# Attention scores from rounded parts: three single-pass products on row halves in place of one fp32 product, the first pair of heads left as it was

## The reference, cut to what matters

```python
# q, k, v: (4, 8, 1152, 64) fp32; w_in: (512, 2048), w_out: (2048, 512), alpha: (2048,)
q_pool = q.reshape(B, H, S // 2, 2, D).mean(axis=3)          # 576 queries a head
scores = scale * np.matmul(q_pool, k.transpose(0, 1, 3, 2))  # 576 x 1152
scores = scores - np.max(scores, axis=-1, keepdims=True)
attn = np.exp(scores)
attn = attn / (np.sum(attn, axis=-1, keepdims=True) + 1e-09)
out = np.matmul(attn, v)
...
x = out.transpose(0, 2, 1, 3).reshape(B * S, H * D)          # 2304 x 512
h = x @ w_in
g = np.maximum(h, 0.0) + alpha * np.minimum(h, 0.0)
return g @ w_out
```

## Time and profile before

| | us |
|---|---|
| median of 3 runs | 889.04 (888.99 to 889.9) |
| the profiled execution | 888.61 |
| span of its core, first to last instruction | 886.8 |

### The profile page before, as it was taken

One profiled execution on the slowest core, in us unless ns is written; L12 is line 12 of the kernel. 1 busy time (PEld: TensorE's weight loads), 2 busy tenths in 40 slices (PEclk: granted clock), 3 DMA queues, 4 the chain that ended last, 5 costly groups with the idle time before them and its releaser, 6 DMA issues. The chain is left out here.

```text
span 886.8 us, 20078 instructions
## 1 busy us (share of the span) xinstructions
PE 861.6 (97%) x6631; PEld 618.1 (70%) x6631; DVE 514.7 (58%) x792; ACT 422.4 (48%) x935; POOL 204.8 (23%) x170
## 2 busy tenths in 40 slices
PE   8899999999999999999999999999999999999997
PEld 5455555555555555555557999998999998999996
DVE  4677777777777777777674344444434445444443
ACT  3666666666666666666663222225222224222222
POOL 3101111110101111110403322333223323233230
PEclk9999999999999999999999999999999999999999
DMA  8725644464435634464122212123222222321211
GB/s 196 174 58 135 152 94 115 97 152 116 122 95 125 152 94 111 101 152 113 48 86 69 60 59 71 59 60 107 84 70 61 59 66 88 109 59 59 63 43 72
DMA packets 42670, 84.37 MB, mean 95 GB/s; under 512 B 7568, under 2 KB 15760, under 8 KB 42640
## 3 DMA queue, kind: packets, MB, share of 16 engines
q1 hardware_dynamic: 40640, 80.06, 35.2%
q10 hardware_dynamic: 2000, 3.93, 1.3%
HBM read 79.18 MB, written 4.79 MB: 95 GB/s over the span
## 5 line engine op out<-in xcount | busy, mean ns | idle before, releaser
L763 PE MATMUL slot_ps<-ff 128*128 128x384 f32 x1152 | 217.8, 337 | 1.4 <-PEq L760 1.4
L763 PEld LDWEIGHTS slot_ps<-ff 128*128 128x128 f32 x1152 | 204.3, 188 | 11.1 <-issue 3.3
L546 DVE TENSOR_REDUCE neg_max<-s_ps 128x1 f32<-128x1152 f32 x144 | 194.7, 1352 | 18.1 <-DVEq L545 17.4
L779 PE MATMUL s_ps<-ff 128*128 128x512 f32 x720 | 182.3, 394 | 1.7 <-PEq L777 1.3
L677 PE MATMUL s_ps<-k_f,q_f 64*128 64x512 f32 (+1 forms) x640 | 159.2, 620 | 1.3 <-PEq L729 1.1
L443 ACT ACTIVATE e_sb<-s_ps,neg_max 128x1024 f32<-128x1024 f32 x144 | 159.6, 1109 | 0.0
L710 PE MATMUL pv_ps<-pt,v_f 128*64 128x256 f32 (+1 forms) x1152 | 155.1, 412 | 0.2 <-PEq L729 0.2
L779 PEld LDWEIGHTS s_ps<-ff 128*128 128x128 f32 x720 | 133.4, 188 | 26.0 <-issue 3.0
L710 PEld LDWEIGHTS pv_ps<-pt,v_f 128*64 128x64 f32 x1152 | 76.7, 136 | 95.9 <-issue 52.6
L598 DVE TENSOR_SCALAR e_sb<-slot_ps,alpha_sb 128x384 f32<-128x384 f32 x96 | 59.3, 617 | 113.2 <-DVEq L596 113.2
L580 DVE COPY pt<-slot_ps 128x512 f32<-128x512 f32 x144 | 98.6, 685 | 39.1 <-DVEq L579 39.1
(11 more groups left out here) (47 smaller groups left out, 525.6 us busy)
## 6 DMA issues: line engine op xcount, KB each, us to landing
k_f<-in_k SPq DMA_DIRECT2D x64, 288.0 KB, 4.2
q_raw<-in_q SPq DMA_DIRECT2D x62, 288.0 KB, 4.1
wi_raw<-in_w_in SPq DMA_DIRECT2D x48, 256.0 KB, 2.6
wo_raw<-in_w_out SPq DMA_DIRECT2D x48, 256.0 KB, 2.6
v_f<-in_v SPq DMA_DIRECT2D x32, 288.0 KB, 3.7
out<-pt ACTq DMA_DIRECT2D x5, 768.0 KB, 4.1
inv_bc<-sums SPq DMA_DIRECT2D x32, 80.0 KB, 3.7
k_end<-in_k SPq DMA_DIRECT2D x64, 32.0 KB, 3.9
```

The costliest lines, as they stand in the source:

```text
L546: nc.vector.tensor_reduce(out=neg_max[:, b:b + 1], in_=s_ps[:, S_AT[b]:S_AT[b] + NKEY], op=ALU.max, axis=AX_X, negate=True).then_inc(max_r ...
L763: ins = nc.tensor.matmul(slot_ps[h][:, 0:TOK], w[i][:, d * P:(d + 1) * P], x[h][:, d * TOK:(d + 1) * TOK], start=(d == 0 and w is wi_hi an ...
L779: ins = nc.tensor.matmul(y_ps[h][t], g[h][:, t * P:(t + 1) * P], w[i], start=(first == 0 and j == 0), stop=(last == 1 and j == 2))
```

## The change

From the second pair of heads on, the large scores are made as the feed-forward products are: q and k are each split into a rounded part and the rest, and the scores are the sum of q_hi k_hi, q_hi k_lo and q_lo k_hi, accumulated in PSUM, each product again as two matmuls on the two row halves. The mixed tile has six such products: the queries get 64 columns of zeros, put in on the host (`with_gaps`), so that 128 columns of the first head end in zeros and 128 of the second begin with them, and both add up in one tile. The small scores stay fp32. The first pair of heads keeps the fp32 scores (`first_scores`); its raw q and k lie at the end of `x_f`, in the part that is written last.

k no longer goes straight into its place: it is loaded into one raw buffer, and GpSimd makes from it k_hi, k_lo and k_end, and from q the pooled q_f, q_hi and q_lo. The parts of even pairs and of odd pairs are two halves of one tensor `kq`, which also takes the place of `ff` in the feed-forward half; so GpSimd waits for the last release of the even set before it splits x. A pair's buffers are released by one semaphore, `qk_free`. SyncE's queue has another order.

```diff
-                for h, first, m, to in SOURCE[t]:
...
             def big_scores(s):
 
-                t, b, g = s % TILES, s % 2, s // TILES % 2
+                b, g = s % 2, s // TILES % 2
+                terms = []
+                for h, col in WIDE[s % TILES]:
+                    i = 2 * g + h
+                    terms += [(q_hi[i], k_hi[i], col), (q_hi[i], k_lo[i], col), (q_lo[i], k_hi[i], col)]
+                pieces = [None, None]
+                for j, (qp, kp, col) in enumerate(terms):
+                    for row, at in enumerate(BIG[b]):
+                        rows = slice(row * HALF, (row + 1) * HALF)
+                        pieces[row] = nc.tensor.matmul(s_ps[:, S_AT[b] + at:S_AT[b] + at + BANK],
+                                                       qp[rows, col:col + P], kp[rows, at:at + BANK],
+                                                       start=(j == 0), stop=(j == len(terms) - 1))
+                return pieces
...
-                    for ins in big_scores(s + 2):
+                    for ins in first_scores(s + 2) if s + 2 < TILES else big_scores(s + 2):
                         ins.then_inc(s_ready, 1)
...
+            def split_q(i, raw, done):
...
+                nc.gpsimd.tensor_copy(q_hi[i], q_f[i][:, :]).then_inc(pool_self, 1)
+                pool.wait_ge(pool_self, 1).then_inc(pool_self, -1)
+                nc.gpsimd.tensor_tensor(q_lo[i], q_f[i][:, :], q_hi[i].bitcast(F32),
+                                        ALU.subtract).then_inc(pool_self, 1)
...
+            def split_qk(i):
+                split_q(i, q_raw, q_raw_in)
                 pool.sem_inc(q_raw_free, 1)
...
+                pool.wait_ge(k_raw_in, 32).then_inc(k_raw_in, -32)
+                nc.gpsimd.tensor_copy(k_hi[i], k_raw[:, :]).then_inc(pool_self, 1)
+                pool.wait_ge(pool_self, 1).then_inc(pool_self, -1)
+                nc.gpsimd.tensor_tensor(k_lo[i], k_raw[:, :], k_hi[i].bitcast(F32), ALU.subtract).then_inc(pool_self, 1)
+                pool.wait_ge(pool_self, 1).then_inc(pool_self, -1)
+                nc.gpsimd.tensor_copy(k_end[i][0:D, :, :], key_ends(k_raw[0:D, :])).then_inc(pool_self, 1)
+                pool.wait_ge(pool_self, 1).then_inc(pool_self, -1)
+                pool.sem_inc(k_ready[i], 1)
+                pool.sem_inc(k_raw_free, 1)
+
+            def split_pair(g):
+                pool.wait_ge(qk_free[g], 1).then_inc(qk_free[g], -1)
+                split_qk(2 * g), split_qk(2 * g + 1)
...
             pool.wait_ge(x_done, NPAIR - 2)
+            pool.wait_ge(qk_free[0], 1).then_inc(qk_free[0], -1)
...
             with sp.Fori(0, NPAIR // 2 - 2) as two:
                 for g in range(2):
 
-                    sums_and_qk(two * 2 + 3 + g, 1 - g)
+                    store_sums(0), spread_sums(0)
+                    load_q_raw(two * 4 + 7 + 2 * g)
+                    store_sums(1)
+                    load_k_raw(two * 4 + 7 + 2 * g)
+                    spread_sums(1)
                     load_v_pair(two * 2 + 2 + g, g)
+                    load_qk(two * 4 + 8 + 2 * g)
...
+    def with_gaps(a):
+
+        gap = np.zeros(a[0::2].shape[:3] + (P // 2,), a.dtype)
+        first, second = a[0::2], a[1::2]
+        both = np.stack((np.concatenate((first[..., :320], gap, first[..., 320:]), axis=3),
+                         np.concatenate((gap, second), axis=3)), axis=1)
+        return both.reshape((a.shape[0],) + both.shape[2:])
```

More of the change, by code:

```diff
@@ L127, in build @@
                 [s_ps[:, 3 * BANK:4 * BANK], s_ps[:, 4 * BANK:5 * BANK], pv_ps[:, :]]]
-        k_in = [sem(f"k{i}_in") for i in range(4)]
+        k_raw_in = sem("k_raw_in")
+        q_raw_in = sem("q_raw_in")
         k_upper_in = [sem(f"k{i}_upper_in") for i in range(2)]
@@ L147, in build @@
         q_ready = [sem(f"q{i}_ready") for i in range(4)]
+        k_ready = [sem(f"k{i}_ready") for i in range(4)]
         pool_self = sem("pool_self")
@@ L663, in small_scores @@
                 rows = UPPER if s < 4 else slice(0, P)
-                for h, first, m, to in SOURCE[t]:
+                for h, col, m, to in SOURCE[t]:
                     ins = nc.tensor.matmul(s_ps[to:to + m, S_AT[b] + at:S_AT[b] + at + P],
-                                           q_f[2 * g + h][rows, first:first + m], k_end[2 * g + h][rows, end, :],
+                                           q_f[2 * g + h][rows, col:col + m], k_end[2 * g + h][rows, end, :],
                                            start=True, stop=True)
@@ L675, in big_scores @@
                     rows = slice(row * HALF, (row + 1) * HALF) if s > 1 else UPPER
-                    for h, first, m, to in SOURCE[t]:
+                    for h, col, m, to in SOURCE[s]:
                         ins = nc.tensor.matmul(s_ps[to:to + m, S_AT[b] + at:S_AT[b] + at + BANK],
-                                               q_f[2 * g + h][rows, first:first + m],
-                                               k_f[2 * g + h][rows, at:at + BANK], start=True, stop=True)
+                                               q_f[h][rows, col:col + m], k_first[h][rows, at:at + BANK],
+                                               start=True, stop=True)
                     pieces.append(ins)
@@ L692, in begin_scores @@
                     i = 2 * g + t
-                    pe.wait_ge(k_in[i], 64).then_inc(k_in[i], -64)
+                    pe.wait_ge(k_ready[i], 1).then_inc(k_ready[i], -1)
                     pe.wait_ge(q_ready[i], 1).then_inc(q_ready[i], -1)
@@ L797, in _ @@
             small_scores(0).then_inc(bank2_ready, 1)
-            for ins in big_scores(0):
+            for ins in first_scores(0):
                 ins.then_inc(s_ready, 1)
@@ L801, in _ @@
             begin_scores(1)
-            for ins in big_scores(1):
+            for ins in first_scores(1):
                 ins.then_inc(s_ready, 1)
```

148 lines of the change are left out of this document (78 added, 70 removed).

## The result

| | before | after |
|---|---|---|
| median, us | 889.1 (888.99 to 889.9, 4 runs) | 893.36 (893.22 to 893.66, 4 runs) |
| span of the profiled core, us | 886.8 | 891.5 |

The changed kernel is slower: 1.0049 times the time of before, 95% interval 1.0036 to 1.0061. The forecast was 888.7, no change that can be measured; the range of 881 to 903 holds the time.

A forecast was written before the change was run, and what follows sets the result against it. TensorE, 97% busy, was taken to bound only four of nine attention stretches, waiting for the ring in the others. Bursts -1.7, first tiles +0.2 and VectorE holds +1.2 gave -0.3: 888.7 us against 889.04, range 881 to 903.

The forecast's parts named there:

- SyncE's queue: Loads and stores of sums: a store slipping by a microsecond leaves reciprocals wanted only 12 us after it; cost nothing.
- 0 to 3 us; I take 0: GpSimd's work at the start, before the burst of step 8: if late, a one-time cost; taken as 0.
- Rival 4: GpSimd or a transfer is late for a head, each pair, needing 6 us more than reckoned; 895; chance 0.04.
- Bursts: TensorE's large scores: plain bursts fall from 1.01 to 0.85 us, mixed ones rise from 1.02 and 1.24 to 1.55.
- rival 3: TensorE's pair of passes is dearer than 0.232, for instance through unhidden weight loading; 893 to about 912; chance 0.14.
- What reaches the end: Attention loop: shorter bursts count only in four of nine stretches, mixed tiles cost 0.84 a body; net -1.7 us.
- the ring: Attention half: ninth copy, row maximum and cut exponential on VectorE and ScalarE, starting from TensorE's small scores; TensorE waits for it.
- VectorE against GpSimd: Invert of group 1 meets GpSimd's rounding of k, waiting 0.1 to 0.2 us; half of +2.4 taken, +1.2.
- Rival 2: Group 1's invert meets GpSimd's subtraction of k, holding VectorE up to 2.6 us once a pair; 922; chance 0.08.
- GpSimd: Seven instructions a head in place of two, 21 to 22 us a pair; hidden, by 6 us.
- The start: GpSimd's and VectorE's q work on the first tiles grows by 64 columns; +0.2 us.

The follow-up runs named there:

- Experiments 1 to 3: Changed kernel with the second group's store earlier (891.36 us); with it one transfer later (900.54); the first of these with even heads' k loads also behind the store (888.48).
- experiment 5: Changed kernel with the second group's store earlier, its large scores made from the rounded parts' product alone; 895.10 us, ratio 1.0081.
- experiment 8: Changed kernel with four raw k buffers, SyncE's queue ordered as before the change, and mixed-tile scores in fp32; 933.61 us, ratio 1.0530.
- experiment 3: Changed kernel with the second group's store earlier and each even head's k load moved behind the first group's store; 888.48 us, ratio 0.9995.
- experiment 2: Changed kernel with the second group's store put one transfer later, behind the load of head 6's q; 900.54 us, ratio 1.0126.

## Why the prediction was wrong, point by point

**The step that failed is "SyncE's queue", its "Nothing" for the store of the sums.** It looked at the loop, where the store is due 22 us after the release and the reciprocals have 12 us in hand, and not at the instructions ahead of the loop, where two heads' loads stand in front of the same store and each k waits for GpSimd. There the store slipped not by a microsecond but by 9.5, and with the 7.7 us of the way through DRAM (55.47 to 63.22) that is more than the 14 until VectorE is ready for the reciprocals (45.97 to 60.11). Experiments 1 to 3 give it its price: by the profile 3.4 us of waiting and 2.1 of a lower clock at the first place; by the medians 2.0 for the first alone and 2.9 more for the second, which takes the first one's place once that is gone; 4.9 in all. The clue was in the diff and in the prediction's own numbers: two heads are 21 us of GpSimd, and the line `load_qk(4), load_qk(5)` stands ahead of `store_sums(1)`. The prediction reckoned GpSimd's lateness at the start ("0 to 3 us; I take 0") only as far as the burst of step 8 that needs the parts, not as far as the loads, and what is queued behind them. Rival 4 named a late GpSimd or transfer, each pair, at 895; it came once, and cost nearly as much.

**Bursts.** Forecast 0.85 and 1.55, measured 0.87 and 1.57 to 1.59. The pair of passes came out as forecast, 0.23 for 0.232: the second to the fifth pair of a mixed burst start 0.69 apart. What the prediction had too small, by some 0.02, is the fixed part for filling and changing over, 0.155. The two row halves run side by side, and rival 3 falls. The Trainium skill's page "TensorE: Matmul & The Clock Gate", Part 3, says that a load overlaps running matmuls only when the row group differs. The trace is at odds with it: from 226.50 on each weight load (0.18) starts with the matmul of its own half and is done before the next pair, 0.23 later.

**What reaches the end.** Forecast -1.7 us for 7.5 bodies, -0.23 a body; measured -0.22 a body over the six from step 34 to 142. The split under it holds in its direction: over the same six bodies the kernel with fp32 mixed tiles gains 4.5 us more than the one beside it, 0.75 a body, where the longer mixed bursts are 0.9 and the prediction charged 0.84. That leaves 0.97 a body that the plain bursts save, of 16 x 0.14 = 2.2: under half, where the prediction's -1.7 us holds 1.07. So added length cost some 0.8 of itself and removed length gave back 0.4; that a longer burst pushes the ring where a shorter one waits for it is a reading of these two numbers that no run tests by itself.

**Luck in the total.** With the two places repaired the kernel stands at -0.7 against the kernel before, near the forecast of -0.3, but partly by chance: the forecast holds +1.2 for holds of VectorE in the loop that cost nothing, and leaves out what the start costs, below.

**VectorE against GpSimd.** The prediction took +1.2 for an invert that would have to wait 0.1 to 0.2 in the rounding of k. The phase came out as reckoned, within 0.1: in the changed kernel's loop the sum starts 0.06 to 0.14 before the rounding ends. The cost was nothing: a held sum ends some 0.02 after GpSimd's instruction, and one that starts 0.13 or less before that end is done by then in its usual 0.15. Rival 2 did not happen but its mechanism is shown, at up to its price: 2.25 us in experiment 5, at the invert of group 1 that it named, and 2.43 in experiment 8, at the invert of group 0, because GpSimd was late and not early. The sum of row_sum ends with GpSimd's instruction, whether that has two inputs (1.14, 2.43) or one (0.64). The Trainium skill's page "SBUF — State Buffer", in the section on the two separate sides, has an exclusive lock in both directions, and the trace agrees with this rule; the prediction's doubt whether VectorE could be held is settled.

**GpSimd** takes from 215.04 to 236.04 for a pair, 21.0, as reckoned.

**The start.** Forecast +0.2, measured +0.5 at step 1 (17.14 against 16.61), but the other kernels with the same start, experiment 3's among them, were 0.0 to 0.9 late there in their profiled executions. Whether the change costs anything in these first steps stays open.

**The first pass through the ring.** From the start of step 10 to that of step 12 the changed kernel loses 0.87, which is in the 0.8 of step 14 and was not in the sum. Half of it is the first mixed tile in the new form: step 11 costs 0.43 in the changed kernel and in every run with the same bursts, and nothing in the two with fp32 mixed tiles. The rest, 0.44 in step 10, is for the most part VectorE held ahead of the loop, where the prediction looked for no such wait:

```profile
45.07 0.42 DVE L606 SCALAR_TENSOR_TENSOR sum_eps<-row_sum 128x4 f32<-128x4 f32 x1
```

```profile
43.93 1.55 POOL L391 TENSOR_TENSOR q_raw<-q_raw 128x640 f32<-128x640 f32 x1 [3.90 <-POOLq L390]
```

The sum lasts 0.27 too long. In experiment 3's kernel the same one lasts 1.08, and step 10 loses 1.10; with four buffers for raw k it is not held, and step 10 loses 0.16.

## What to carry to other kernels

When a load gets a new condition, walk the queue that issues it from its first instruction, not only through the loop's steady state: ahead of the loop the consumers are not yet in phase, and one wait in the wrong place costs once what no later step gives back. After a gap is closed, look again at the next one behind it; it may have been hidden by the first. In a kernel that is bound by a ring through several engines, price longer and shorter work apart: here what was added to a burst counted for some 0.8 of its length and what was taken away for less than half. And when less work gives no less time, look on the other engines for an instruction that lasts longer than it did.

## What the runs showed of the hardware

- VectorE's scalar_tensor_tensor on 128x4 with both inputs in SBUF waits for a running GpSimd instruction to end, also when that has one input: 1.14 and 0.64 us for what takes 0.15 alone. A VectorE reciprocal with one input did not wait (0.18), and a sum that began 0.08 before GpSimd's end still took 0.15.
- With one product in place of two the time rose from 882.96 to 895.10: TensorE's gaps of 1.7 to 3.9 us came behind held sums of 0.98 to 3.19, and the granted clock fell behind five of the eight, to 0.50 behind the longest two. Gaps of nearly one length differ in this: behind those of 1.8 that end at 163.31 and 219.48 the clock fell, behind those that end at 108.00, 335.55 and 390.64 it stayed at 1.00.
- After an idle gap of 3.2 us the clock stayed at 0.50 in the rows of the next five us, all of it work, and then came back; that cost 2.1 us more on top of the gap, and 2.0 behind the gap of 10.4 us of experiment 2.
- A pair of fp32r passes over 512 columns, one on each row half, takes 0.23 us, as one such pass on the whole array did in the feed-forward half (0.232).
